# Squares of the last stage on ScalarE, an input mixed in place four quads earlier, and VectorE's sums ahead of its preparation steps

## The chip, the cores and the metric

One core of a Trainium2 chip. The metric is the device time of one execution in microseconds, median of several runs; lower is better. The engines are TensorE (PE in the profile), VectorE (DVE), ScalarE (ACT), GpSimd (POOL) and SyncE (SP), which here only issues DMAs. Each works through its own instructions in order and waits on semaphores.

## The reference

Three layers over a batch of 2, a sequence of 768 and a width of 512, in fp32. The first is a windowed attention with block summaries. The other two are these:

```python
# second layer
xt = x.transpose(0, 2, 1)
h = np.maximum(xt @ w_tok1, 0.0) @ w_tok2
u = x + h.transpose(0, 2, 1)
x = u + np.maximum(u @ w_ch1, 0.0) @ w_ch2      # w_ch1: 512 x 1536
# third layer (the last stage of the kernel)
x_prev = x shifted by one row of the sequence, zeros first
xk = mu_k * x + (1.0 - mu_k) * x_prev
xr = mu_r * x + (1.0 - mu_r) * x_prev
k = np.maximum(xk @ w_k, 0.0)                    # w_k: 512 x 1024
v = k * k @ w_v
r = 1.0 / (1.0 + np.exp(-(xr @ w_r)))
out = r * v
```

## The kernel before, in words

Each fp32 factor is split into a high part (fp32r) and a low part, the rest; three matmuls (high x high, high x low, low x high) make one product (`three`, L1311 to L1313). The high part is a copy by ScalarE or GpSimd, the low part a subtraction by VectorE or GpSimd. Activations lie transposed in `u`: four tiles of 128 channels, and per batch one zero column and 768 columns, so that `x_prev` is the same tile read one column earlier (`u_tile(kk, g, 1)`).

**Quads.** The channel products are cut into quads of 256 x 256 blocks of the weight and two halves (384 columns) of the sequence, done with seven products in place of eight (`PRODUCTS`, in the order P1, P6, P2, P7, P5, P4, P3) on sums and differences of the blocks of the weight (`w1S`, by GpSimd) and of the activation (`ucF`). There are 20 quads: 0 to 5 and 6 to 11 for the two batches of the second layer (`quad`), 12 to 15 and 16 to 19 for the two batches of the last stage (`quad_k`). A set is the activation of one batch and layer; set 3 feeds quads 16 to 19.

**PE** runs for quad q: P1, two value tiles of quad q-1, P6, one tile, P2, two, P7, one, P5, two, P4, two, P3, two (`TILE_GAPS`; a value tile is k*k @ w_v for 128 rows). The first value tile needs the low part of R21 of quad q-1, the seventh that of R12. P1 waits until all five sums of the quad before are done and its weights are split; P7 waits for the sum of P6, P4 for that of P7, P3 for that of P5.

**VectorE** makes five sums per quad (`plus`, L1177: P6 into u2, P7 into u3, P5 into c22, P4 into c21, P3 into c12), the squares (L1194 for `kr`, L1181 for the other three: max with 0, times itself), the low parts of the results (`low_k`, L1187) and of the next quad's weights (`low_w1`, L997, L1000 and L1003), and what `ahead(q, place)` lists for one of three places in the quad. **ScalarE** turns out P1 (`p1`, L812), relu of P2 (`kr`, L818), the high parts of the weights (`high_w1`), of the results (`high_k`, L809), and its share of `ahead`. **GpSimd** makes the sums of weights (L568 to L573, waiting for the last product of the quad before), splits w_v (L578, L582) and the low part of w_r (L587).

**What `ahead` does** is written out by hand in tables, keyed by quad and place: `T_AT` and `U_AT` make the sums and the high (L716) and low parts of the next set, `MIX_AT` mixes xk, `XR_AT` mixes xr (ScalarE (1 - mu) * x_prev, L751, then VectorE adds mu * x, L1075), `XR_HIGH_AT` and `XR_LOW_AT` split it (L757, L1082). A mix or split works on 128 x 384.

**The gates.** After the products of quad 16, PE computes xr @ w_r for batch 0 in six tiles (`gate(0)`), after quad 19 that of batch 1; ScalarE applies the sigmoid (L838), VectorE multiplies by v (L1234). The gate's first three tiles need the low parts of xr tiles 0 to 3, the others those of 4 to 7, and `wait_piece` both halves of w_r.

## Time and profile before

| | |
|---|---|
| median of 3 runs | 509.79 us (508.15 to 510.85) |
| profiled execution | 510.17 us, its span 508.4 us |
| mean granted clock of TensorE | 0.977 of full speed |
| busy: PE, PEld, DVE, ACT, POOL | 92%, 82%, 70%, 45%, 43% of the span |
| chain that ended last | PE 69%, DVE 15%, ACT 7%, idle issue 5% |

The span runs from the first to the last instruction; the time of a run holds 1.77 us more. Times in rows are microseconds from the span's start. A row of a timeline is one instruction (or a few alike, with their count), in brackets how long its engine stood idle before it and what released it. A row of windows gives the busy time in one stretch and TensorE's mean granted clock there, 1.00 for 2.4 GHz and 0.50 for 1.2 GHz.

### The profile page before, as it was taken

To read this page: it belongs to the slowest core of one execution; us is meant where nothing else is said; L and a number is where in the kernel's file an instruction comes from. 1 tells how busy PE (TensorE), PEld (TensorE's weight loads), DVE (VectorE), ACT (ScalarE), POOL (GpSimd) and SP (SyncE) were. 2 spreads that over 40 slices of the span, in tenths; PEclk is the share of its full clock that TensorE was granted. 3 is DMA by queue.
4 is the path that set the end of the run, shared out by engine and by line. 5 is a ranking of instruction groups with operands and counts; after the bars stand their busy time and mean duration, and the time that the engine had idled before them with its cause. 6 is when DMAs were issued, how large, how long until landed. Compare 5 with 4: busy or idle time off the path is not lost.

```text
span 508.4 us, 7788 instructions
## 1 busy us (share of the span) xinstructions
PE 466.3 (92%) x2848; PEld 415.3 (82%) x2848; DVE 354.1 (70%) x732; ACT 228.9 (45%) x473; POOL 220.9 (43%) x213
## 2 busy tenths in 40 slices
PE   5789889999999999999999999697898759989997
PEld 4677778889999999999998998586787648878885
DVE  6589996496766565567676863876987993699503
ACT  6699996464333333334433343161264542552120
POOL 6647765422534566433564346516245290063000
PEclk9899999999999999999999999998989959999999
DMA  6999944311121121221212212112020312210003
GB/s 183 244 227 224 197 94 81 111 41 43 42 85 58 67 84 41 84 79 46 85 44 81 63 62 83 43 43 77 8 82 1 124 41 104 104 43 0 2 0 124
DMA packets 45441, 41.20 MB, mean 81 GB/s; under 512 B 20832, under 2 KB 36704, under 8 KB 45408
## 3 DMA queue, kind: packets, MB, share of 16 engines
q1 hardware_dynamic: 45408, 40.78, 29.5%
q8 instruction: 19, 0.31, 0.3%
q14 instruction: 14, 0.11, 0.1%
HBM read 37.62 MB, written 3.15 MB: 80 GB/s over the span
## 4 chain that ended last, share of the span: by engine, by line
PE 69%; DVE 15%; ACT 7%; issue 5%; DMA 2%; POOL 2%; SPq 0%; ACTq 0%; DVEq 0%; POOLq 0%
PE bank L1311 16%; PE bank L1312 15%; PE bank L1313 15%; PE bank L1448 12%; PE bank L1449 6%; ACT e_sb L638 3%; DVE rL L1187 2%; DMA v<-in_v_dram 2%; DVE xrL L1082 2%; DVE c L1181 2%; DVE w1L L1003 2%; ACT qbd L618 1%; PE bank L1291 1%; DVE c L1177 1%; PE bank L1363 1%
## 5 line engine op out<-in xcount | busy, mean ns | idle before, releaser
L1311 PE MATMUL bank<-ucH,w1H 128*128 128x384 f32 x280 | 96.1, 343 | 13.7 <-DVE c L1177 8.5
L1313 PE MATMUL bank<-ucH,w1L 128*128 128x384 f32 x280 | 95.0, 339 | 0.0
L1312 PE MATMUL bank<-ucL,w1H 128*128 128x384 f32 x280 | 94.9, 339 | 0.0
L568 POOL TENSOR_TENSOR w1S<-stg 128x256 f32<-128x256 f32 x20 | 19.8, 991 | 168.9 <-PE bank L1313 168.9
L1311 PEld LDWEIGHTS bank<-ucH,w1H 128*128 128x128 f32 x280 | 53.2, 190 | 22.6 <-issue 15.6
L582 POOL TENSOR_TENSOR w2L<-stg,w2H 128x512 fp32r<-128x512 f32 x40 | 60.2, 1526 | 1.6
L1312 PEld LDWEIGHTS bank<-ucL,w1H 128*128 128x128 f32 x280 | 53.6, 191 | 2.0
L1313 PEld LDWEIGHTS bank<-ucH,w1L 128*128 128x128 f32 x280 | 53.3, 190 | 0.0
L774 ACT ACTIVATE rH<-c 128x384 fp32r<-128x384 f32 x36 | 18.9, 526 | 68.4 <-DVE c L1115 68.4
L809 ACT ACTIVATE rH<-c 128x384 fp32r<-128x384 f32 x24 | 12.6, 525 | 61.2 <-DVE c L1181 61.2
L1312 PE MATMUL bank<-w2L,rH 128*128 128x512 f32 x96 | 38.8, 404 | 0.0
L1311 PE MATMUL bank<-w2H,rH 128*128 128x512 f32 x96 | 38.7, 404 | 0.0
L1313 PE MATMUL bank<-w2H,rL 128*128 128x512 f32 x96 | 38.6, 402 | 0.0
L1448 PE MATMUL bank<-rL,w2H 128*128 128x512 f32 x96 | 37.6, 392 | 0.0
L1448 PE MATMUL bank<-rH,w2L 128*128 128x512 f32 x96 | 37.6, 392 | 0.0
L1448 PE MATMUL bank<-rH,w2H 128*128 128x512 f32 x96 | 37.6, 392 | 0.0
L1115 DVE TENSOR_TENSOR u<-bank,p 128x384 f32<-128x384 f32 x24 | 13.4, 557 | 33.1 <-PE bank L1313 33.0
L578 POOL CAST w2H<-stg 128x1024 fp32r<-128x1024 f32 x20 | 21.9, 1096 | 28.9 <-PE bank L1313 25.3
L1120 DVE SCALAR_TENSOR_TENSOR rL<-c,rH 128x384 fp32r<-128x384 f32 x36 | 23.7, 659 | 13.6 <-ACT rH L774 13.6
L638 ACT ACTIVATE e_sb<-s_sb,nmx 128x120 f32<-128x120 f32 x96 | 29.8, 384 | 0.8 <-DVE nmx L902 0.8
L1311 PE MATMUL bank<-WrH,xrH 128*128 128x512 f32 x48 | 19.8, 411 | 9.3 <-DVE xrL L1082 9.3
L1449 PE MATMUL bank<-rH,w2L 128*128 128x256 f32 x96 | 27.0, 281 | 0.0
(142 smaller groups left out, 1187.5 us busy)
## 6 DMA issues: line engine op xcount, KB each, us to landing
stg<-in_moe_w_ch_dram SPq DMA_DIRECT2D x24, 512.0 KB, 3.5
stg<-in_moe_w_k_dram SPq DMA_DIRECT2D x8, 512.0 KB, 3.5
stg<-in_moe_w_v_dram SPq DMA_DIRECT2D x8, 512.0 KB, 3.4
vw<-in_v_dram SPq DMA_DIRECT2D x16, 240.0 KB, 5.6
kn<-in_k_dram SPq DMA_DIRECT2D x8, 384.0 KB, 5.6
qn<-in_q_dram SPq DMA_DIRECT2D x8, 384.0 KB, 6.7
v<-in_v_dram SPq DMA_DIRECT2D x8, 384.0 KB, 5.6
stg<-in_moe_w_tok_dram SPq DMA_DIRECT2D x6, 256.0 KB, 3.9
```

Source lines behind the costliest of these rows:

```text
L568: pool.tensor_tensor(s1, a21, a22, ALU.add).then_inc(w1s_done, 1)
L578: pool.tensor_copy(hi, stg[2][:, :]).then_inc(wb_high, 1)
L582: pool.tensor_tensor(lo[:, part], stg[2][:, part], hi[:, part].bitcast(F32), ALU.subtract).then_inc(wb_split, 1)
L638: act.activation(e_sb[par][:, n, :], s_sb[r][:, n, :], ACT.Exp, bias=nmx[:, r, n:n + 1], scale=-1.0).then_inc(exp_done, 1)
L774: act.activation(rH[slot][:, f, half * GR:half * GR + GR], src, func).then_inc(rh_done, 1)
L1115: dve.tensor_tensor(dst[:, :], acc, other[:, :], ALU.add).then_inc(sum_done, 1)
L1120: dve.scalar_tensor_tensor(out=rL[slot][:, f, half * GR:half * GR + GR], in0=src, scalar=0.0, in1=hi.bitcast(F32), op0=ALU.max, op1=ALU.su ...
L1311: pe.matmul(dst, wH, mH, start=start, stop=False, **more)
L1312: pe.matmul(dst, wH, mL, start=False, stop=False, **more)
L1313: return pe.matmul(dst, wL, mH, start=False, stop=stop, **more)
L1448: pe.matmul(wide, w, r[slot][:, f, 0:512], start=begin, stop=end, skip_group_check=True)
L1449: ins = pe.matmul(side, w, r[slot][:, f, 512:S], start=begin and d % 2 == 0, stop=end, skip_group_check=True)
```

## The change

In the last stage the squares go from VectorE to ScalarE. `kr` is squared by an ACTIVATE in place right after its relu, and its high part is made next, ahead of `high_w1`. For R22, R21 and R12 a new `power` waits for VectorE's sum, then does Relu in place, waits for that, and does Square in place; `high_k` follows. VectorE's `square` and its product for `kr` are gone.

xr of batch 0 is mixed in quads 8 to 11, one of its eight tiles at each of places 1 and 2, half 1 of the sequence first. It overwrites `u`, which nothing else needs by then; ScalarE's part goes through the two buffers `sg`. Its splits follow in quad 16, one or two tiles per place, the last four after it. For batch 1 mixes and splits go one per place in quads 17 to 19. `MIX_AT` of quad 13 and `U_AT` of quads 14 and 15 are spread over more places.

In VectorE's `quad_k` the order changes: `low_w1` part 0 ahead of `low_k(R11)`, P4's sum ahead of `low_k(R22)`, P3's sum ahead of `low_k(R21)`, place 3 ahead of `low_k(R12)`.

```diff
--- before.py
+++ after.py
@@ -220,7 +220,7 @@
         tk_mixed, xk_mixed = sem("tk_mixed"), sem("xk_mixed")
         tr_mixed, xr_mixed = sem("tr_mixed"), sem("xr_mixed")
         xrh_done, xrl_done = sem("xrh_done"), sem("xrl_done")
-        kr_done, sq_done, v_done, tile_done = sem("kr_done"), sem("sq_done"), sem("v_done"), sem("tile_done")
+        kr_done, relu_done, sq_done, v_done, tile_done = sem("kr_done"), sem("relu_done"), sem("sq_done"), sem("v_done"), sem("tile_done")
         wr_done, sg_done, o_done = sem("wr_done"), sem("sg_done"), sem("o_done")
         ld_out = [sem("ld_out0"), sem("ld_out1"), sem("ld_out2")]
 
@@ -312,13 +312,17 @@
                 (9, 1): (3, 4), (9, 2): (5, 6), (14, 1): (3, 4), (14, 2): (5, 6)}
         U_AT = {(1, 1): (0,), (2, 1): (1,), (3, 1): (3,), (4, 1): (4,), (4, 2): (5,), (5, 1): (6,), (5, 2): (2,),
                 (10, 1): (0, 1), (10, 2): (3,), (11, 1): (4, 5), (11, 2): (6, 2),
-                (14, 3): (0, 1), (15, 1): (3, 4), (15, 2): (5, 6), (15, 3): (2,)}
+                (14, 3): (0,), (15, 1): (1, 3), (15, 2): (4, 5), (15, 3): (6, 2)}
 
         MIX_AT = {(7, 1): ((0, 0), (1, 0)), (7, 2): ((2, 0), (3, 0)), (8, 1): ((0, 1), (1, 1)), (8, 2): ((2, 1), (3, 1)),
-                  (13, 1): ((0, 0), (1, 0), (2, 0), (3, 0)), (13, 2): ((0, 1), (1, 1), (2, 1), (3, 1))}
-        XR_AT = {(16, 1): (0, 1), (16, 2): (2, 3), (17, 1): (0, 1), (17, 2): (2, 3), (18, 1): (4, 5), (18, 2): (6, 7)}
-        XR_HIGH_AT = {(16, 2): (0, 1), (16, 3): (2, 3), (17, 2): (0, 1), (17, 3): (2, 3), (18, 2): (4, 5), (18, 3): (6, 7)}
-        XR_LOW_AT = {(16, 3): (0, 1, 2, 3), (17, 3): (0, 1, 2, 3), (18, 3): (4, 5, 6, 7)}
+                  (13, 1): ((0, 0), (1, 0), (2, 0)), (13, 2): ((3, 0), (0, 1), (1, 1)), (13, 3): ((2, 1), (3, 1))}
+
+        XR_ORDER = (4, 5, 6, 7, 0, 1, 2, 3)
+        XR_AT = {(8, 1): (4,), (8, 2): (5,), (9, 1): (6,), (9, 2): (7,), (10, 1): (0,), (10, 2): (1,), (11, 1): (2,),
+                 (11, 2): (3,), (17, 1): (0,), (17, 2): (1,), (17, 3): (2,), (18, 1): (3,), (18, 2): (4,), (18, 3): (5,),
+                 (19, 1): (6,), (19, 2): (7,)}
+        XR_SPLIT_AT = {(16, 1): (0,), (16, 2): (1, 2), (16, 3): (3,), (17, 2): (0,), (17, 3): (1,), (18, 1): (2,),
+                       (18, 2): (3,), (18, 3): (4,), (19, 1): (5,), (19, 2): (6,), (19, 3): (7,)}
 
         def set_ahead(q):
             return 1 if q < NFP else 2 if q < NQ else 3
@@ -748,13 +752,21 @@
 
             def mix_r(b, n):
                 kk, half = n % KT, n // KT
-                act.activation(xrF[:, kk, half * GR:half * GR + GR], u_tile(kk, 2 * b + half, 1), ACT.Copy,
+                if b == 0:
+                    i = XR_ORDER.index(n)
+                    if i >= 2:
+                        act.wait_ge(xr_mixed, i - 1)
+                    dst = sg[i % 2][:, 0:GR]
+                else:
+                    dst = xrF[:, kk, half * GR:half * GR + GR]
+                act.activation(dst, u_tile(kk, 2 * b + half, 1), ACT.Copy,
                                scale=omu[:, 1, kk:kk + 1]).then_inc(tr_mixed, 1)
 
             def high_xr(b, n):
                 kk, half = n % KT, n // KT
-                act.wait_ge(xr_mixed, 8 * b + n + 1)
-                act.activation(xrH[:, kk, half * GR:half * GR + GR], xrF[:, kk, half * GR:half * GR + GR],
+                part = slice(half * GR, half * GR + GR)
+                act.wait_ge(xr_mixed, 8 if b == 0 else 8 + n + 1)
+                act.activation(xrH[:, kk, part], u_tile(kk, half) if b == 0 else xrF[:, kk, part],
                                ACT.Copy).then_inc(xrh_done, 1)
 
             def ahead(q, place):
@@ -764,7 +776,7 @@
                     high_u(set_ahead(q), i)
                 for n in XR_AT.get((q, place), ()):
                     mix_r(q // 17, n)
-                for n in XR_HIGH_AT.get((q, place), ()):
+                for n in XR_SPLIT_AT.get((q, place), ()):
                     high_xr(q // 17, n)
 
             def quad(q):
@@ -804,9 +816,16 @@
 
                 slot, done, k = q % 2, NPROD * q, q - NQ
 
-                def high_k(n, f, half, src):
+                def high_k(n, f, half, c):
                     act.wait_ge(sq_done, 4 * k + n)
-                    act.activation(rH[slot][:, f, half * GR:half * GR + GR], src[:, :], ACT.Copy).then_inc(rh_done, 1)
+                    act.activation(rH[slot][:, f, half * GR:half * GR + GR], c[:, :], ACT.Copy).then_inc(rh_done, 1)
+
+                def power(n, c):
+
+                    act.wait_ge(sum_done, 5 * q + n + 1)
+                    act.activation(c[:, :], c[:, :], ACT.Relu).then_inc(relu_done, 1)
+                    act.wait_ge(relu_done, 3 * k + n - 1)
+                    act.activation(c[:, :], c[:, :], ACT.Square).then_inc(sq_done, 1)
 
                 act.wait_ge(prod_done, done + P1)
                 act.activation(p1[:, :], bank[0][:, 0:GR], ACT.Copy).then_inc(p1_done, 1)
@@ -816,15 +835,20 @@
                 act.wait_ge(prod_done, done + P2)
                 act.wait_ge(rl_done, 4 * (q - 1) + R11)
                 act.activation(kr[:, :], bank[0][:, 0:GR], ACT.Relu).then_inc(kr_done, 1)
+                wait_second(act, q - 2)
+                act.wait_ge(kr_done, k + 1)
+                act.activation(kr[:, :], kr[:, :], ACT.Square).then_inc(sq_done, 1)
+                high_k(R11, 0, 0, kr)
                 if q < NA - 1:
                     high_w1(q + 1)
-                wait_second(act, q - 2)
-                high_k(R11, 0, 0, kr)
                 ahead(q, 2)
+                power(R22, c22)
                 high_k(R22, 1, 1, c22)
                 if q == 16:
                     high_wr(1)
+                power(R21, c21)
                 high_k(R21, 1, 0, c21)
+                power(R12, c12)
                 high_k(R12, 0, 1, c12)
                 ahead(q, 3)
 
@@ -849,8 +873,6 @@
                     act.wait_ge(x2_done, 6 * B)
                 quad_k(q)
                 if q == NQ + NKP:
-                    for n in range(KT, 2 * KT):
-                        mix_r(0, n)
                     for n in range(KT, 2 * KT):
                         high_xr(0, n)
                     gates(0)
@@ -1070,17 +1092,23 @@
 
             def mix_r(b, n):
                 kk, half = n % KT, n // KT
-                dst = xrF[:, kk, half * GR:half * GR + GR]
-                dve.wait_ge(tr_mixed, 8 * b + n + 1)
-                dve.scalar_tensor_tensor(out=dst, in0=u_tile(kk, 2 * b + half), scalar=mu[:, 1, kk:kk + 1], in1=dst,
+                x = u_tile(kk, 2 * b + half)
+                if b == 0:
+                    i = XR_ORDER.index(n)
+                    dst, part = x, sg[i % 2][:, 0:GR]
+                else:
+                    i, dst = n, xrF[:, kk, half * GR:half * GR + GR]
+                    part = dst
+                dve.wait_ge(tr_mixed, 8 * b + i + 1)
+                dve.scalar_tensor_tensor(out=dst, in0=x, scalar=mu[:, 1, kk:kk + 1], in1=part,
                                          op0=ALU.mult, op1=ALU.add).then_inc(xr_mixed, 1)
 
             def low_xr(b, n):
                 kk, half = n % KT, n // KT
                 part = slice(half * GR, half * GR + GR)
                 dve.wait_ge(xrh_done, 8 * b + n + 1)
-                dve.tensor_tensor(xrL[:, kk, part], xrF[:, kk, part], xrH[:, kk, part].bitcast(F32),
-                                  ALU.subtract).then_inc(xrl_done, 1)
+                dve.tensor_tensor(xrL[:, kk, part], u_tile(kk, half) if b == 0 else xrF[:, kk, part],
+                                  xrH[:, kk, part].bitcast(F32), ALU.subtract).then_inc(xrl_done, 1)
 
             def ahead(q, place):
                 for kk, half in MIX_AT.get((q, place), ()):
@@ -1091,7 +1119,7 @@
                     low_u(set_ahead(q), i)
                 for n in XR_AT.get((q, place), ()):
                     mix_r(q // 17, n)
-                for n in XR_LOW_AT.get((q, place), ()):
+                for n in XR_SPLIT_AT.get((q, place), ()):
                     low_xr(q // 17, n)
 
             def wide(b, d):
@@ -1176,11 +1204,6 @@
                     dve.wait_ge(prod_done, done + n)
                     dve.tensor_tensor(dst[:, :], acc, other[:, :], ALU.add).then_inc(sum_done, 1)
 
-                def square(n, c):
-                    dve.wait_ge(sum_done, 5 * q + n + 1)
-                    dve.scalar_tensor_tensor(out=c[:, :], in0=c[:, :], scalar=0.0, in1=c[:, :], op0=ALU.max,
-                                             op1=ALU.mult).then_inc(sq_done, 1)
-
                 def low_k(n, f, half, src):
                     hi = rH[slot][:, f, half * GR:half * GR + GR]
                     dve.wait_ge(rh_done, 4 * q + n)
@@ -1190,38 +1213,33 @@
                 dve.wait_ge(p1_done, q + 1)
                 dve.wait_ge(sum_done, 5 * q)
                 plus(P6, u2, Bk, p1)
-                dve.wait_ge(kr_done, k + 1)
-                dve.tensor_tensor(kr[:, :], kr[:, :], kr[:, :], ALU.mult).then_inc(sq_done, 1)
                 ahead(q, 1)
                 if q == NQ:
                     wide(1, 0)
                 plus(P7, u3, Bk, p1)
-                low_k(R11, 0, 0, kr)
                 if q < NA - 1:
                     low_w1(q + 1, 0)
+                low_k(R11, 0, 0, kr)
                 dve.wait_ge(sum_done, 5 * q + 2)
                 dve.wait_ge(rl_done, 4 * q)
                 plus(P5, c22, A, u3)
-                square(R22, c22)
                 ahead(q, 2)
                 if q == NQ:
                     wide(1, 1)
+                plus(P4, c21, Bk, p1)
                 low_k(R22, 1, 1, c22)
-                plus(P4, c21, Bk, p1)
-                square(R21, c21)
                 if q < NA - 1:
                     low_w1(q + 1, 1)
-                low_k(R21, 1, 0, c21)
                 if q == NQ:
                     side(1, 1)
                 plus(P3, c12, A, u2)
-                square(R12, c12)
-                low_k(R12, 0, 1, c12)
+                low_k(R21, 1, 0, c21)
                 if q == NQ:
                     wide(1, 2)
                     wide(1, 3)
                     side(1, 3)
                 ahead(q, 3)
+                low_k(R12, 0, 1, c12)
 
             def outputs(b):
                 for st in range(NT):
@@ -1242,8 +1260,6 @@
                     dve.wait_ge(x2_done, 6 * B)
                 quad_k(q)
                 if q == NQ + NKP:
-                    for n in range(KT, 2 * KT):
-                        mix_r(0, n)
                     for n in range(KT, 2 * KT):
                         low_xr(0, n)
                     outputs(0)
```

## Rows read from the trace of the kernel before

**Rows 1.** Windows: length, busy PE PEld DVE ACT POOL, clock, DMA

```profile
308.20:328.70 20.50, 16.14 (x90) 14.60 (x91) 11.37 (x19) 4.65 (x9) 10.09 (x10) 1.00 0.18 58
328.70:349.30 20.60, 17.45 (x79) 15.39 (x79) 17.05 (x28) 8.79 (x17) 7.80 (x8) 0.91 0.13 45
349.30:369.00 19.70, 17.41 (x79) 15.35 (x79) 13.59 (x21) 4.74 (x9) 7.59 (x6) 0.92 0.17 53
369.00:387.70 18.70, 17.43 (x78) 15.17 (x78) 17.27 (x23) 9.03 (x15) 8.00 (x6) 0.91 0.16 53
387.70:413.00 25.30, 15.96 (x79) 14.06 (x79) 21.12 (x28) 13.48 (x25) 13.63 (x11) 0.88 0.25 83
413.00:431.50 18.50, 18.50 (x73) 15.10 (x74) 11.03 (x13) 6.37 (x10) 5.68 (x5) 0.88 0.17 65
431.50:447.20 15.70, 15.70 (x80) 13.91 (x78) 10.63 (x20) 7.67 (x15) 1.20 (x2) 1.00 0.26 93
447.20:464.50 17.30, 16.02 (x79) 13.86 (x79) 16.61 (x25) 8.43 (x17) 7.00 (x6) 1.00 0.09 31
```

**Rows 2.** Timeline of PE (start, us; idle before, releaser), quads 12, 13

```profile
320.22 0.41 PE L1311 MATMUL bank<-ucH,w1H 128*128 128x384 f32 x1 [1.34 <-DVE u L1177]
...
328.73 0.66 PE L1311 MATMUL bank<-ucH,w1H 128*128 128x384 f32 x1 [3.05 <-DVE c L1177]
```

**Rows 3.** Timeline of DVE, end of quad 13

```profile
344.37 0.55 DVE L1177 TENSOR_TENSOR c<-bank,p 128x384 f32<-128x384 f32 x1
344.95 1.04 DVE L1181 SCALAR_TENSOR_TENSOR c<-c 128x384 f32<-128x384 f32 x1
345.92 1.75 DVE L1003 TENSOR_TENSOR w1L<-w1S,w1H 128x1024 fp32r<-128x1024 f32 x1
347.59 1.07 DVE L1187 TENSOR_TENSOR rL<-c,rH 128x384 fp32r<-128x384 f32 x1
348.58 0.54 DVE L1177 TENSOR_TENSOR c<-bank,u 128x384 f32<-128x384 f32 x1
```

**Rows 4.** Timeline of POOL, same stretch

```profile
346.54 1.71 POOL L571 TENSOR_TENSOR w1S<-w1S,stg 128x256 f32<-128x256 f32 x1
```

**Rows 5.** Timelines of DVE, ACT, DVE, POOL in quad 17

```profile
435.25 0.56 DVE L1177 TENSOR_TENSOR u<-bank,p 128x384 f32<-128x384 f32 x1 [2.21 <-PE bank L1313]
...
436.89 0.49 ACT L818 ACTIVATE kr<-bank 128x384 f32<-128x384 f32 x1 [2.68 <-PE bank L1313]
...
444.38 0.56 DVE L1181 SCALAR_TENSOR_TENSOR c<-c 128x384 f32<-128x384 f32 x1
...
446.00 1.15 POOL L568 TENSOR_TENSOR w1S<-stg 128x256 f32<-128x256 f32 x1 [27.16 <-PE bank L1313]
```

**Rows 6.** Groups by line on ACT (busy, mean ns | idle before)

```profile
L716 ACT ACTIVATE ucH<-ucF 128x768 fp32r<-128x768 f32 x22 | 17.7, 836 | 3.3 <-DVE u L1040 3.1
...
L809 ACT ACTIVATE rH<-c 128x384 fp32r<-128x384 f32 x24 | 12.6, 525 | 61.2 <-DVE c L1181 61.2
...
L751 ACT ACTIVATE xrF<-u,omu 128x384 f32<-128x384 f32 x16 | 8.8, 602 | 0.0
...
L838 ACT ACT_TABLE_LOAD x1 | 1.3, 1283 | 0.0
```

**Rows 7.** Timelines of POOL and DVE, quad 16 and behind it

```profile
400.30 2.40 POOL L587 TENSOR_TENSOR WrL<-stg,WrH 128x1024 fp32r<-128x1024 f32 x1 [6.97 <-ACT WrH L724]
...
400.75 2.37 DVE L1181 SCALAR_TENSOR_TENSOR c<-c 128x384 f32<-128x384 f32 x1
...
407.67 5.14 DVE L1082 TENSOR_TENSOR xrL<-xrF,xrH 128x384 fp32r<-128x384 f32 x4
```

**Rows 8.** Timelines of DVE and PE, end of quad 9

```profile
273.28 1.22 DVE L1003 TENSOR_TENSOR w1L<-w1S,w1H 128x1024 fp32r<-128x1024 f32 x1
274.41 1.11 DVE L1120 SCALAR_TENSOR_TENSOR rL<-c,rH 128x384 fp32r<-128x384 f32 x1
...
276.13 0.41 PE L1311 MATMUL bank<-ucH,w1H 128*128 128x384 f32 x1 [0.76 <-DVE c L1115]
```

## Prediction

> **What bounds the kernel now.** I read the windows of the last stage first, one window from the start of one quad's products to the next [rows 1]: in this program TensorE is the bound, and the question is where it isn't fed. Quad 17 is the clean one: 15.70 us, PE busy in all of it, clock 1.00. Every other quad of the stage should take the same, and takes more: 20.50 (12), 20.60 (13), 19.70 (14), 18.70 (15), 25.30 (16, to the gate), 17.30 (18). The gate of batch 0 takes 18.50 at a mean clock of 0.88.
>
> The timeline of PE shows the holes [rows 2]: PE stands still 1.34 us inside quad 12 and 3.05 us before the first product of quad 13. The others come from [rows 1], length less PE's busy time: 3.15 before quad 14, 2.29 before 15, 1.27 before 16, 9.3 before the gate (25.30 - 15.96) and 1.3 in quad 18 (17.30 - 16.02). There is a second loss: in quads 13 to 15 PE is busy 17.4 us for 15.7 us of work, at a mean clock of 0.91 to 0.92. After the holes of 3.05, 3.15, 2.29 and 9.3 us the clock drops to its half level (1.2 GHz) for a while; after those of 1.34, 1.27 and 1.3 it doesn't. So a long hole costs its length and some 1.6 us more.
>
> What PE waits for is named in [rows 2]: `c` of L1177, VectorE's sum `plus(P3, c12)`. The timeline of DVE at the end of quad 13 [rows 3] shows why it is late: between the sum of P4 (344.37) and that of P3 (348.58) stand a square of 1.04, `low_w1` part 1 of 1.75 and `low_k(R21)` of 1.07. In this stretch GpSimd works [rows 4], and the two inputs from SBUF make DVE's operations wait for it: without GpSimd `low_w1` part 1 takes 1.22 [rows 8] and the square 0.56 [rows 5].
>
> For the clocking of a quad I use quad 17 [rows 5]: its first product starts at 431.45 (431.5 in [rows 1]); P6's sum starts at +3.80, P2's relu at +5.44, and GpSimd, which waits for P3, at +14.55. Between P6 and P2 stands one value tile: 5.44 - 3.80 = 1.64 for a product and a tile. From P2 to P3 come three products with two tiles and one with one, so two tiles and a product take (14.55 - 5.44 - 1.64) / 3 = 2.49. P7, P5, P4, P3 end at +7.9, 9.6, 12.1, 14.5, and the next quad wants c12 at about +15.6.
>
> **Part 1: squares to ScalarE.** DVE loses four operations per quad, 0.56 each [rows 5], more where one waits for GpSimd (1.04 in [rows 3]): 2.2 us or more. ACT gains seven: four squares and three relus (the relu of `kr` exists). No Square runs before; the nearest row is ACT's copy of the same tile, 525 ns [rows 6]; bounds are 0.49 (the relu from PSUM [rows 5]) and 0.60 (L751, with a pointer operand). No row has an ACT operation that waits for the one before it on ACT; DVE's `plus` to square is 0.58 from start to start in [rows 3] for a sum of 0.55, so I take 0.03 for the wait: 0.56 each, 3.9 per quad. ACT's queue per quad becomes: p 0.4, kr with square and copy 1.6, `high_w1` 1.8, three times relu, square, copy 1.65 = 5.0, in sum 8.8; with 8 mixes of 0.55 (8.8 over 16) in quad 13 13.2; with 6 high parts of u (17.7 over 22, 0.8 each) in quad 15 13.6, of 15.7 [rows 6]. It holds.
>
> The new queue, quad 13, offsets from its first product. ACT: p, three mixes to 3.2; kr 5.44 to 7.0; `high_w1` to 8.75; mixes to 10.3; R22 (c22 is there at 10.4) to 12.1; R21 (c21 at 12.7) to 14.4; R12 (c12 at 15.15) to 16.8; two mixes to 17.8. DVE: P6 4.3, mixes 5.9, P7 8.4, w1 part 0 9.4, R11 9.85, P5 10.35, mixes 11.95, P4 12.6, R22 13.1, w1 part 1 14.25 (GpSimd starts at 14.55, so the price is the clean 1.22), P3 14.55 to 15.1. That is before 15.6: no hole. Late instead are R12 and the mixes behind it, done at about +18.9; its reader, the seventh value tile of the next quad, comes at +25. R21's reader, the first value tile, comes at +16.8, and R21 is low at 15.6 to 16.2: half a microsecond of cover; that is what is late next.
>
> **Part 2: order of sums and preparation.** The high and low parts of set 3 are spread (14.3 to 15.3), so quad 15 has six. There GpSimd stands against DVE until +7 and I get P4's sum at 14.1 instead of 12.6, P3's at 16.2 to 16.8: a hole of 0.9, quad 15 16.6 us (bounds 15.7 and 17.7). Quad 12 keeps its 1.34, since `wide(1, 0)` still stands ahead of P7's sum. After it, counted from P4's start at 320.22 [rows 2]: `wide(1, 1)` waits for the chunk behind P4 (+2.4, at 322.6, 0.6 us), P4's sum ends at 323.7, R22 at 324.2, w1 part 1 at 325.4 to 325.9, `side(1, 1)` at 326.5, P3's sum at about 327; the square of 0.5 to 1 us and `low_k(R21)` of 1.07 that stood there are gone. Quad 13 starts at 326.9 instead of 328.7. The hole is 1.2, of the size after which the clock stayed. Quad 12: 18.7.
>
> **Part 3: xr of batch 0 in quads 8 to 11.** This takes eight mixes out of quad 16 and the stretch after it. Before, the gate's first tile waited for four `low_xr` of 5.14 us together, behind `low_k(R12)` and behind squares of which one took 2.37 while GpSimd's `WrL` (2.40) ran [rows 7]. After, three of four are done inside the quad. The last waits: c12 at 15.15 to 17.1 (as GpSimd's second `WrL` goes after or before w1 part 1), R12 on ACT 1.7, `high_xr(3)` 0.4, `low_xr(3)` 0.55: the gate starts at 17.9 to 19.8; I take 19.0 for 25.3. A hole of 3 us remains, hence the half clock for one stretch: the gate's work is 18.5 x 0.88 = 16.3 at full clock, I take 17.9 (bounds 16.3 and 18.5). Batch 1: mixes and splits go one per place; the four `low_xr` that stood ahead of P6's sum in quad 18 are gone: 15.7 for 17.3.
>
> The price is in quads 8 to 11: one mix (some 0.55 on ACT and on DVE, like their other operations on 384 columns) at two places each. Behind place 1 DVE waits for P7 anyway. Place 2 stands ahead of the sums of P4 and P3, and DVE is at the edge there: before quad 10 PE already stands 0.76, behind a `low_r(R21)` of 1.11 for 0.55 [rows 8]. Pushed by half a microsecond, w1 part 1 also slides under GpSimd. I count 0.55, 0.8, 0.4 and 0.75: 2.5 us lost (bounds 0.5, if a wait for GpSimd absorbs the mix, and 4.2, if each adds one more GpSimd operation of about 1 us at two of them). No DMA moves: SP waits for the same splits, at nearly the same offsets.
>
> **Sum**, quads 12, 13, 14, 15, 16, gate, 17, 18: before 20.5 + 20.6 + 19.7 + 18.7 + 25.3 + 18.5 + 15.7 + 17.3 = 156.3; after 18.7 + 15.7 + 15.7 + 16.6 + 19.0 + 17.9 + 15.7 + 15.7 = 135.0. That is 21.3 less, 2.5 back: 18.8. The profiled execution took 510.17 for a span of 508.4, so 491.4; that execution lies 0.4 above the median of the runs, 509.79: 491.0. Own range by the bounds: 2.0 + 0.9 + 1.1 + 1.6 down gives 485.4; 1.7 + 1.1 + 0.8 + 0.6, and 1.6 for a clock that falls before quad 13, gives 496.8 up.
>
> **A rule against it.** The rows say: relu and multiply cost VectorE one operation of 0.56 [rows 5], ScalarE two of about 0.53 [rows 6]. The Trainium skill (ScalarE: Activation LUTs, Rules for kernel authors) puts relu and mul on VectorE, not ScalarE. By that rule the move loses; the trace agrees with it on engine time, but ACT is busy 4.7 to 9.0 us of quads 13 to 15 and DVE 13.6 to 17.3 [rows 1].
>
> **Rivals.**
> 1. The longer chain takes the sum's place. DVE is in order, and `low_k(R22)`, which now waits for three ACT steps, stands ahead of w1 part 1 and of P3's sum. There is 0.5 us between ACT's 12.1 and DVE's 12.6, and 0.3 more before P3. For it: ACT comes out of its mixes only at 10.3, when c22 is there. If a square with its wait costs 1 us more than I take, quads 13 to 16 lose some 1 to 1.5 us each with half clock after one or two: 8 us of the gain gone, 499 (497 to 503). Chance 0.15.
> 2. On the other side: Square and Relu (or Copy) are in different tables. A load takes 1.28 us [rows 6]. With two loads per square, 8 x 1.28 = 10.3 per quad on ACT, 13.6 + 10.3 = 23.9 for a quad of 15.7: 8.2 x 8 = 66 us on top of 491, some 555. It decides once ACT's queue is 18.8 / 8 = 2.4 longer than 15.7, 4.5 us above 13.6: four loads per quad. Against it: Exp, Sigmoid, Relu and Copy run with two loads in all, one of them before the first Exp. Chance 0.03.
> 3. The engine-time rule above as a mechanism: ACT gains 3.9 where DVE loses 2.2; if that chain set the quad's length, 1.7 x 8 = 14 us slower than 510, 524. It needs the first value tile to wait for R21 in all quads. Against it: R21 has 0.5 us of cover. Chance 0.02.
> 4. The change doesn't reach the holes, because the quads 8 to 11 and contention with GpSimd give the gain back: DVE is busy 13.6 to 17.3 us of quads 13 to 15 now and keeps 11 of them. Two waits for GpSimd per quad at 1 us each, 500 to 508 with the clock. Chance 0.05.
>
> **Chances.** Forecast 0.75, the others as given. The range takes in the forecast's own 485.4 to 496.8 and reaches to rival 1's 499 and a little: 484.5 to 500.5. A run here can tell 0.5% (2.5 us) from no change. Faster: 0.75 + 0.15 + 0.04 = 0.94; within 0.5% 0.01; slower 0.05.
>
> **What would show it.** Right: first products of quads 14 to 16 with no hole of over 1 us; clock 1.00 from quad 13 to 16; the gate's hole about 3 us, released by `xrL`; DVE's sum of P3 directly behind `w1L`; ACT in rows relu, square, copy of about 0.53 without idle between them; one table load besides the first. New holes of 0.5 to 1.5 us before quads 9 to 12. Wrong: the value line waiting for rL, a Square of another duration than a copy, table loads in the stage, or the clock at half where PE was fed.

## The result and the profile after

The changed kernel takes 488.48 us (median of 4 runs, 486.57 to 489.74), the kernel before 509.49 in the same comparison: a ratio of 0.9584, 95% interval 0.9543 to 0.9625. Forecast were 491.0 in a range of 484.5 to 500.5. The profiled execution of the changed kernel is its fastest run, 486.57, with a span of 484.8 us. One of the ten runs of a1 below took 758.54 us at a mean clock of 0.562 and is left out of its ratio.

Windows of the changed kernel from one quad's first product to the next one's, for quads 12 to 16, the gate of batch 0, and quads 17 and 18. The columns are those of [rows 1]: start and end, length, busy time of PE, PEld, DVE, ACT, POOL (instructions), granted clock, DMA.

```profile
309.20:328.10 18.90, 16.12 (x90) 14.62 (x90) 8.84 (x15) 7.54 (x15) 8.06 (x8) 1.00 0.17 55
328.10:343.90 15.80, 15.76 (x78) 14.17 (x79) 13.86 (x22) 12.01 (x24) 6.03 (x7) 1.00 0.22 72
343.90:359.60 15.70, 15.70 (x80) 14.05 (x79) 13.92 (x19) 9.29 (x18) 7.58 (x8) 1.00 0.18 62
359.60:375.30 15.70, 15.70 (x80) 14.07 (x79) 13.74 (x18) 12.30 (x23) 8.50 (x8) 1.00 0.22 67
375.30:393.10 17.80, 15.80 (x79) 13.84 (x78) 13.74 (x19) 15.01 (x28) 8.11 (x5) 1.00 0.19 62
393.10:409.60 16.50, 16.47 (x72) 13.55 (x73) 5.68 (x10) 5.22 (x9) 10.00 (x10) 1.00 0.40 133
409.60:425.30 15.70, 15.70 (x79) 14.07 (x78) 8.52 (x15) 9.54 (x19) 1.12 (x2) 1.00 0.27 94
425.30:441.00 15.70, 15.70 (x79) 14.05 (x78) 12.51 (x19) 11.22 (x23) 6.44 (x6) 1.00 0.09 34
```

Against [rows 1]: quads 13, 14, 15 and 18 are at the clean length with PE busy throughout; the clock is 1.00 in every window. ACT's busy time in quad 13 has risen from 8.79 to 12.01 of 15.8, DVE's fell from 17.05 of 20.6 to 13.86. What is left of the holes, in PE's timeline:

```profile
275.85 0.41 PE L1327 MATMUL bank<-ucH,w1H 128*128 128x384 f32 x1 [1.44 <-DVE c L1143]
...
309.24 0.41 PE L1327 MATMUL bank<-ucH,w1H 128*128 128x384 f32 x1 [1.39 <-issue]
...
321.25 0.41 PE L1327 MATMUL bank<-ucH,w1H 128*128 128x384 f32 x1 [1.34 <-DVE u L1205]
...
328.14 0.41 PE L1327 MATMUL bank<-ucH,w1H 128*128 128x384 f32 x1 [1.44 <-DVE c L1205]
...
393.13 0.47 PE L1327 MATMUL bank<-WrH,xrH 128*128 128x512 f32 x1 [2.02 <-DVE xrL L1110]
```

The first two (before quads 10 and 12) were 0.76 [rows 8] and 0.52 and have grown by 0.68 and 0.87 us: the price of the mixes in quads 8 to 11. The gate's hole is 2.02 us in place of 9.3. DVE at the end of quad 13, where [rows 3] had 4.2 us from the sum of P4 to that of P3:

```profile
340.27 0.56 DVE L1205 TENSOR_TENSOR c<-bank,p 128x384 f32<-128x384 f32 x1 [0.17 <-PE bank L1329]
340.75 0.55 DVE L1210 TENSOR_TENSOR rL<-c,rH 128x384 fp32r<-128x384 f32 x1
341.21 1.22 DVE L1025 TENSOR_TENSOR w1L<-w1S,w1H 128x1024 fp32r<-128x1024 f32 x1
342.71 0.56 DVE L1205 TENSOR_TENSOR c<-bank,u 128x384 f32<-128x384 f32 x1 [0.28 <-PE bank L1329]
```

Both sums now wait for PE, and `w1L` takes its clean 1.22: it is done at 342.43, and GpSimd starts at 342.76. And the chain on ACT for R21, three steps that follow one another:

```profile
340.87 0.53 ACT L826 ACTIVATE c<-c 128x384 f32<-128x384 f32 x1 [0.67 <-DVE c L1205]
341.42 0.53 ACT L828 ACTIVATE c<-c 128x384 f32<-128x384 f32 x1
341.98 0.53 ACT L821 ACTIVATE rH<-c 128x384 fp32r<-128x384 f32 x1
```

A Square lasts as long as a copy, and from start to start 0.55 to 0.56 us.

### The profile page after: what moved, and what is told of

The parts are those of the page before. It is cut to its first block, busy times and chain, and to the rows that moved or that the text cites. A ratio compares the mean times of both kernels' runs of the same rounds, so it can differ in the third digit from the quotient of the medians.

```text
span 484.8 us, 7812 instructions
## 1 busy us (share of the span) xinstructions
PE 459.0 (95%) x2848; PEld 410.3 (85%) x2848; DVE 331.2 (68%) x700; ACT 258.2 (53%) x529; POOL 217.3 (45%) x213
## 4 chain that ended last, share of the span: by engine, by line
PE 74%; ACT 9%; DVE 6%; issue 5%; DMA 2%; POOL 2%; SPq 0%; ACTq 0%; DVEq 0%; POOLq 0%
PE bank L1327 18%; PE bank L1329 18%; PE bank L1328 18%; PE bank L1464 12%; PE bank L1465 6%; ACT e_sb L642 4%; DMA v<-in_v_dram 2%; ACT qbd L622 2%; DVE ucF L1056 1%; ACT kt L630 1%; DVE w1L L1025 1%; POOL xL L546 1%; DVE rL L1148 1%; DVE c L1143 1%; PE bank L1397 1%
## 5 line engine op out<-in xcount | busy, mean ns | idle before, releaser
L1327 PE MATMUL bank<-ucH,w1H 128*128 128x384 f32 x280 | 94.7, 338 | 6.0 <-DVE c L1143 1.7
L1329 PE MATMUL bank<-ucH,w1L 128*128 128x384 f32 x280 | 94.0, 336 | 0.0
L572 POOL TENSOR_TENSOR w1S<-stg 128x256 f32<-128x256 f32 x20 | 17.9, 894 | 148.7 <-PE bank L1329 148.7
L586 POOL TENSOR_TENSOR w2L<-stg,w2H 128x512 fp32r<-128x512 f32 x40 | 58.9, 1494 | 1.6
L786 ACT ACTIVATE rH<-c 128x384 fp32r<-128x384 f32 x36 | 18.9, 526 | 69.4 <-DVE c L1143 69.4
L582 POOL CAST w2H<-stg 128x1024 fp32r<-128x1024 f32 x20 | 22.8, 1142 | 30.2 <-PE bank L1329 24.3
L1035 DVE TENSOR_TENSOR ucL<-ucF,ucH 128x768 fp32r<-128x768 f32 x22 | 24.9, 1157 | 3.7 <-ACT ucH L720 3.7
L1465 PE MATMUL bank<-rL,w2H 128*128 128x256 f32 x96 | 26.9, 280 | 0.0
```

The costliest lines, as they stand in the source:

```text
L582: pool.tensor_copy(hi, stg[2][:, :]).then_inc(wb_high, 1)
L586: pool.tensor_tensor(lo[:, part], stg[2][:, part], hi[:, part].bitcast(F32), ALU.subtract).then_inc(wb_split, 1)
L786: act.activation(rH[slot][:, f, half * GR:half * GR + GR], src, func).then_inc(rh_done, 1)
L1035: dve.tensor_tensor(ucL[b % 2][:, i, :, :], src, ucH[b % 2][:, i, :, :].bitcast(F32), ALU.subtract).then_inc(ul_done, 1)
L1327: pe.matmul(dst, wH, mH, start=start, stop=False, **more)
L1329: return pe.matmul(dst, wL, mH, start=False, stop=stop, **more)
```

## The experiments

Each was compared with the kernel before on the same chip. The groups a, b and c ran on three chips, on which the kernel before took 509.49, 510.49 and 510.41, so a difference between medians of two groups is uncertain by about 1 us. Firmer are the distances between first products in the profiles: quads 8 to 11 take 64.3 to 64.5 us in every kernel that leaves them as they were or mixes behind P3's sum. The time to the first product of quad 8, ahead of which nothing was changed, is 242.3 to 244.2. The table of distances stands behind the first four.

**a1, VectorE's order alone.** The squares stay where they were, each right behind its sum.

```diff
                 plus(P7, u3, Bk, p1)
-                low_k(R11, 0, 0, kr)
                 if q < NA - 1:
                     low_w1(q + 1, 0)
+                low_k(R11, 0, 0, kr)
...
-                low_k(R22, 1, 1, c22)
                 plus(P4, c21, Bk, p1)
                 square(R21, c21)
+                low_k(R22, 1, 1, c22)
...
-                low_k(R21, 1, 0, c21)
...
                 plus(P3, c12, A, u2)
                 square(R12, c12)
-                low_k(R12, 0, 1, c12)
+                low_k(R21, 1, 0, c21)
...
                 ahead(q, 3)
+                low_k(R12, 0, 1, c12)
```

> The kernel before with VectorE's new order alone; the squares stay on VectorE, each right behind its sum, and the xr tables stay. Theory: the holes before quads 13 to 16 come from what stands between P4's and P3's sum, and taking low_k(R22) and low_k(R21) out of the way is enough for most of them: about 498 us (500 at worst), the 9.3 us hole before the gate stays. Rival (only the four squares taken off VectorE count): 506 or more.

Measured: 507.47 us, ratio 0.9952 (0.9926 to 0.9978). The theory failed: the order alone is worth 2 us (3.0 in the table below), not 11.

**a2, squares alone.** ScalarE's `quad_k` of the changed kernel, VectorE's of before without its squares.

```diff
                 plus(P6, u2, Bk, p1)
-                dve.wait_ge(kr_done, k + 1)
-                dve.tensor_tensor(kr[:, :], kr[:, :], kr[:, :], ALU.mult).then_inc(sq_done, 1)
...
-                square(R22, c22)
...
-                square(R21, c21)
...
-                square(R12, c12)
```

> The kernel before with the squares on ScalarE alone; VectorE's order and the xr tables stay. Theory: VectorE has 0.56 to 1 us less ahead of P3's sum, but low_k(R21) still stands before it and waits for the three steps on ScalarE; holes of under 0.7 us stay, no half clock: about 495 us. Rival 1 of the prediction (the longer chain takes the sum's place): the holes stay at 2 to 3 us, 503 or more.

Measured: 502.01 us, ratio 0.9848 (0.9808 to 0.9887). Between the theory (495) and rival 1 (503), and nearer to the rival.

**a3, xr and the tables.** The changed kernel with the `quad_k` of before on both engines. With xr come the spread `MIX_AT` and `U_AT` of quads 13 to 15; no run parts them from xr.

> The kernel before with xr of batch 0 in place in quads 8 to 11 and the new tables alone; squares and VectorE's order stay. Theory: the gate's hole falls from 9.3 to about 3 us and quad 18 loses its 1.3, quads 8 to 11 cost 2.5, holes before quads 13 to 16 stay: about 504 us. Rival (the price in quads 8 to 11 eats it): 507 or more.

Measured: 503.1 us, ratio 0.9876 (0.9838 to 0.9914). Near the 504 expected, but not by the way expected: the holes before quads 13 to 16 were to stay, and the one before quad 14 fell from 3.13 to 1.07 us. No operation of xr stands in quads 13 to 15 in either kernel, so these quads' 4.9 us come from the spread tables, in part through a half clock that stayed away. The gate's hole is 4.71 us, not 3. PE's timeline before quad 14:

```profile
349.26 0.41 PE L1325 MATMUL bank<-ucH,w1H 128*128 128x384 f32 x1 [1.07 <-DVE c L1193]
```

**a4, squares and order, without xr.** The kernel before with both engines' `quad_k` of the changed one; all tables are those of before.

> The changed kernel without the xr part: squares on ScalarE and VectorE's new order, with the old xr tables. Theory: quads 13 to 16 at 15.7 to 16.6, gate's hole still 5 us or more: about 494 us, that is 5 to 6 above the changed kernel and no more than 2 below squares alone. Rival (the xr part gives nothing): 489.

Measured: 488.04 us, ratio 0.9572 (0.9531 to 0.9613). The rival was right: beside the other two parts, xr and the tables give nothing (the changed kernel 488.48).

Microseconds between first products, worked out from PE's timelines; "gate" is the length of batch 0's gate, "sum" goes from quad 12 to the end of quad 18:

| | 8 to 11 | 12 | 13 | 14 | 15 | 16 | gate | 17 | 18 | sum |
|---|---|---|---|---|---|---|---|---|---|---|
| before | 64.5 | 20.5 | 20.5 | 19.7 | 18.8 | 25.2 | 18.5 | 15.7 | 17.3 | 156.3 |
| a1, order | 64.5 | 20.5 | 20.1 | 18.9 | 17.9 | 24.1 | 18.7 | 15.7 | 17.4 | 153.3 |
| a2, squares | 64.3 | 20.0 | 18.7 | 16.4 | 17.1 | 23.8 | 19.2 | 16.3 | 16.9 | 148.3 |
| a3, xr and tables | 66.8 | 20.5 | 18.5 | 18.4 | 17.2 | 20.6 | 18.7 | 15.7 | 15.9 | 145.6 |
| a4, squares and order | 64.5 | 18.9 | 15.8 | 15.7 | 15.9 | 18.9 | 18.0 | 15.7 | 15.7 | 134.5 |
| changed, all three | 66.9 | 18.9 | 15.8 | 15.7 | 15.7 | 17.9 | 16.5 | 15.7 | 15.7 | 131.8 |

Why the order alone does so little is seen in DVE's timeline of a1 at the end of quad 13 (first product at 328.83):

```profile
344.44 0.55 DVE L1177 TENSOR_TENSOR c<-bank,p 128x384 f32<-128x384 f32 x1
345.02 0.56 DVE L1181 SCALAR_TENSOR_TENSOR c<-c 128x384 f32<-128x384 f32 x1
345.50 1.10 DVE L1187 TENSOR_TENSOR rL<-c,rH 128x384 fp32r<-128x384 f32 x1
346.52 1.74 DVE L1003 TENSOR_TENSOR w1L<-w1S,w1H 128x1024 fp32r<-128x1024 f32 x1
348.19 0.54 DVE L1177 TENSOR_TENSOR c<-bank,u 128x384 f32<-128x384 f32 x1
```

P4's sum itself is late, at +15.6 and without waiting for PE (PE itself is some 1.7 us late here by a stretch at half clock, as in the kernel before: busy 17.45 for 15.70 [rows 1]); in the changed kernel it waits for PE and starts at +12.1. So `w1L` falls into GpSimd's time and takes 1.74 for 1.22. Where the queue falls behind is seen earlier in the same timeline:

```profile
336.80 0.56 DVE L1194 TENSOR_TENSOR kr<-kr 128x384 f32<-128x384 f32 x1 [1.61 <-ACT kr L818]
337.28 2.20 DVE L1068 SCALAR_TENSOR_TENSOR ucF<-u,mu,ucF 128x384 f32<-128x384 f32 x4
339.40 0.55 DVE L1177 TENSOR_TENSOR u<-bank,p 128x384 f32<-128x384 f32 x1
```

VectorE stands idle 1.61 us at the product for `kr`, which needs P2's relu, and the four mixes of place 1 and P7's sum stand behind it. From here on no sum of the quad waits for PE. With the squares on ScalarE the mixes come first and fill that idle time (in the changed kernel P7's sum waits 1.47 us for PE). Whether `ahead(q, 1)` put ahead of the product for `kr`, with all squares left on VectorE, would give part of this was not run. An order can't mend a queue that is behind before the place of the edit, and a1's edit begins behind P7's sum. With the squares alone P7's sum waits for PE (1.41 us) and `w1L` is clean again, and another wait takes over:

```profile
343.21 0.55 DVE L1189 TENSOR_TENSOR c<-bank,p 128x384 f32<-128x384 f32 x1
343.68 1.22 DVE L1015 TENSOR_TENSOR w1L<-w1S,w1H 128x1024 fp32r<-128x1024 f32 x1
345.47 1.12 DVE L1199 TENSOR_TENSOR rL<-c,rH 128x384 fp32r<-128x384 f32 x1 [0.58 <-ACT rH L809]
346.52 0.54 DVE L1189 TENSOR_TENSOR c<-bank,u 128x384 f32<-128x384 f32 x1
```

`low_k(R21)` waits 0.58 us for ACT's third step and then takes 1.12 us for 0.55, with GpSimd at work from 344.66, and P3's sum stands behind it. That is rival 1 of the prediction, in the kernel without the new order. Two more runs split the order.

**c2 and c3, squares and one move of the order.** Cut, against a2:

```diff
c2:
-                low_k(R21, 1, 0, c21)
                 if q == NQ:
                     side(1, 1)
                 plus(P3, c12, A, u2)
+                low_k(R21, 1, 0, c21)
c3:
-                low_k(R22, 1, 1, c22)
                 plus(P4, c21, Bk, p1)
+                low_k(R22, 1, 1, c22)
```

> Squares on ScalarE alone, and of the new order only P3's sum ahead of low_k(R21). Theory: what kept the holes with the squares alone was low_k(R21) waiting in VectorE's queue for ScalarE's three steps, in front of P3's sum; moving that one operation gives nearly all of what the whole order gives: about 489 (487 to 491), against 502 for the squares alone and 488 for the whole order. Rival (P4's sum behind low_k(R22) counts as much): 495.

> Squares on ScalarE alone, and of the new order only P4's sum ahead of low_k(R22). Theory: P4's sum comes half a microsecond earlier and so does R21's chain, but low_k(R21) still waits ahead of P3's sum; most holes stay: 498 to 502. Rival (P4's sum counts as much): 495.

Measured: c2 490.78 us, ratio 0.9600 (0.9560 to 0.9641); c3 498.7, ratio 0.9766 (0.9725 to 0.9808). Of the 14 us between the squares alone (502.0) and the whole order (488.0), moving P3's sum ahead of `low_k(R21)` gives 11.2. Moving P4's alone gives 3.3. These are medians of two chips; from quad 12 to the end of quad 18 the profiles give 10.0 (138.3) and 3.7 (144.6) of 13.8.

**b1, the mixes at place 3.**

```diff
-        XR_AT = {(8, 1): (4,), (8, 2): (5,), (9, 1): (6,), (9, 2): (7,), (10, 1): (0,), (10, 2): (1,), (11, 1): (2,),
-                 (11, 2): (3,),
+        XR_AT = {(8, 3): (4, 5), (9, 3): (6, 7), (10, 3): (0, 1), (11, 3): (2, 3),
```

> The changed kernel with the eight mixes of xr of batch 0 at place 3 of quads 8 to 11, behind P3's sum, two per quad, in place of one at each of places 1 and 2. Theory: the 2.4 us that quads 8 to 11 lost are the mixes' place ahead of P4's and P3's sums, where VectorE has no slack; behind P3's sum it idles 2.4 us. The holes of 1.44 before quad 10 and 1.39 before quad 12 fall to those of the kernel before (0.76, 0.52): 2.4 less than the changed kernel, about 486. Rival (the mixes cost wherever they stand, by contention with GpSimd, which is at work there): no difference, or slower.

Measured: 486.20 us, ratio 0.9521 (0.9491 to 0.9551), 2.3 less than the changed kernel. Quads 8 to 11 take 64.5 again, and the hole before quad 10 is 0.76 as in [rows 8]. The price was the place, not the mixes: the pair there takes long beside GpSimd too (2.40 for two), but no sum stands behind it.

```profile
259.82 2.40 DVE L1103 SCALAR_TENSOR_TENSOR u<-u,mu,sg 128x384 f32<-128x384 f32 x2
```

**b2, the second layer's last additions one sum later.**

```diff
-                if q == NQ:
-                    wide(1, 0)
                 plus(P7, u3, Bk, p1)
...
                 if q == NQ:
-                    wide(1, 1)
+                    wide(1, 0)
                 plus(P4, c21, Bk, p1)
+                if q == NQ:
+                    wide(1, 1)
...
+                plus(P3, c12, A, u2)
                 if q == NQ:
                     side(1, 1)
-                plus(P3, c12, A, u2)
```

> The changed kernel with the additions wide(1,0), wide(1,1) and side(1,1) of quad 12 one sum later each, so that no sum waits behind a second-layer chunk. Theory: the hole of 1.34 before P4 of quad 12 goes, and that of 1.44 before quad 13 falls below 0.5: 2 to 2.5 less than the changed kernel, about 486. Rival (PE waits for something else there, such as the sum of P6 or the splits): under 1 us.

Measured: 485.81 us, ratio 0.9516 (0.9484 to 0.9547), 2.7 less than the changed kernel. Both holes of quad 12 are gone: 15.7 for 18.9. The three moves were made together; of them only `wide(1, 0)` stood ahead of P7's sum, for which P4 waited, while the share of each in the hole before quad 13 is not parted.

**b3, xr tile 3 split at place 2 of quad 16.**

```diff
-        XR_SPLIT_AT = {(16, 1): (0,), (16, 2): (1, 2), (16, 3): (3,),
+        XR_SPLIT_AT = {(16, 1): (0,), (16, 2): (1, 2, 3),
```

> The changed kernel with the split of xr tile 3 at place 2 of quad 16 in place of place 3, so that the gate waits for no step behind R12. Theory: the gate's hole of 2.02 (released by xrL) falls to about 0.7, then set by GpSimd's second WrL; in runs where that hole brings a stretch at half clock, 1.5 more: about 486. Rival (WrL or P3's sum was nearly as late): under 0.5 us.

Measured: 485.81 us, ratio 0.9522 (0.9494 to 0.9550), 2.7 less. The first matmul of the gate:

```profile
391.86 0.50 PE L1327 MATMUL bank<-WrH,xrH 128*128 128x512 f32 x1 [0.68 <-POOL WrL L591]
```

The hole is 0.68, and its releaser is now GpSimd's second `WrL`, as expected: 1.34 us of the 2.7. The rest stays open. Three of the changed kernel's four runs have a mean clock of 0.996, as b1's profiled execution has with one stretch at half clock in the gate (last section). But c1's profiled execution has 0.996 too, and its half clock (0.53 in the window 19.2 to 22.8 us) lies far ahead of the gate.

**b4, each relu of `power` done twice.**

```diff
                     act.activation(c[:, :], c[:, :], ACT.Relu).then_inc(relu_done, 1)
-                    act.wait_ge(relu_done, 3 * k + n - 1)
+                    act.wait_ge(relu_done, 2 * (3 * k + n - 1) - 1)
+                    act.activation(c[:, :], c[:, :], ACT.Relu).then_inc(relu_done, 1)
+                    act.wait_ge(relu_done, 2 * (3 * k + n - 1))
```

> The changed kernel with the relu of R22, R21 and R12 done twice, 0.56 us more on each chain and 1.7 per quad on ScalarE's queue (13.3 us more in the stage); the result is the same. Theory: the chain has about 0.5 us of cover before VectorE reads R22 and R21, so it costs at most 1.5 us in sum: 489 to 490. Rival 1 of the prediction (the chain is what sets the sums): 0.5 to 0.6 per quad and the clock, 493 or more.

Measured: 491.89 us, ratio 0.9629 (0.9593 to 0.9666): 3.4 more than the changed kernel, more than twice the 1.5 I allowed, and less than the rival's 4.5. In the profile quads 12, 14, 16 and 18 are 0.6 to 0.9 longer, 2.8 together, quads 13, 15 and 17 are unchanged, and the gate is 1.5 longer at half clock behind a hole of 2.95. In quad 14 PE waits in the middle of the quad, for the sum of P6, and DVE's timeline shows why:

```profile
347.67 2.94 DVE L1092 SCALAR_TENSOR_TENSOR ucF<-u,mu,ucF 128x384 f32<-128x384 f32 x2 [2.12 <-ACT ucF L750]
350.54 1.65 DVE L1212 TENSOR_TENSOR rL<-c,rH 128x384 fp32r<-128x384 f32 x1
352.10 0.55 DVE L1207 TENSOR_TENSOR u<-bank,p 128x384 f32<-128x384 f32 x1
```

The two mixes of quad 13's place 3 stand on ACT behind the chain for R12; VectorE waits 2.12 us for them, then takes 2.94 us for two mixes and 1.65 for a low part, and the next quad's first sum stands behind them. The cover that ends first is there, not at R21.

**c1, b1 to b3 together.**

> The changed kernel with all three edits that each gained: xr mixes at place 3 of quads 8 to 11, the wide and side additions of quad 12 one sum later, the split of xr tile 3 at place 2 of quad 16. Theory: they touch different holes, so they add: 2.4 + 3.2 + 1.4 by their pitches, and no hole of 2 us is left that could bring the half clock (about 1 us on the median of the changed kernel's runs): about 480.5 (479 to 482). Rival (the holes hide one another, as the parts of the change did): 483 or more.

Measured: 480.65 us (479.75 to 480.98), ratio 0.9402 (0.9372 to 0.9432): 7.8 us less than the changed kernel. The three edits add, since each closes holes that no other touches: in the profiles, from quad 8 to the end of quad 18, 2.4, 3.0 and 1.4 alone (b1's longer gate at half clock left out) and 6.8 together. Its windows for quad 12, quad 16 and the gate:

```profile
308.10:323.80 15.70, 15.70 (x91) 14.63 (x91) 10.22 (x16) 8.43 (x17) 7.51 (x7) 1.00 0.18 61
...
371.10:387.60 16.50, 15.82 (x80) 13.86 (x78) 13.21 (x18) 14.13 (x26) 8.09 (x5) 1.00 0.19 65
387.60:404.10 16.50, 16.50 (x73) 13.62 (x74) 6.13 (x11) 6.10 (x11) 9.99 (x10) 1.00 0.38 135
```

## Why the prediction was right, and where it wasn't

The sum was near and somewhat low: 18.8 us forecast, 21.0 measured between medians, 23.6 between the profiled spans. Of the 23.6, 1.4 lie before quad 8 (its first product at 242.3 for 243.7), where nothing was changed. From quad 8 to the end of quad 18 it is 22.1: quad 15 gave 0.9 more than forecast, quad 16 1.1 and the gate 1.4. The queues of parts 1 and 2 came out as worked out; what part 3 put down to xr in quads 16 and 18 came from the other two parts (6), so the near sum doesn't bear out how it was split.

1. **Part 1, the costs on ScalarE**: right. The new operations last 0.526 us on average (taken 0.53) and 0.56 with their wait. The 0.03 for the wait was too small, though: copies of the same tile that don't wait for one another start 0.41 to 0.42 apart (`xrH` in the kernel before), so the wait takes 0.14 to 0.15 of the queue. No table is loaded for Square: two loads in all, so rival 2 is out. Rival 3, the engine-time rule, needed value tiles that wait for R21; none does in the changed kernel, and it takes 488, not 524. The squares alone (a2) already gain 7.5 us.
2. **Part 1, quads 13 to 15**: 20.6 + 19.7 + 18.7 were to become 15.7 + 15.7 + 16.6 and became 15.8 + 15.7 + 15.7. The step that was too dear is quad 15: I had DVE's P4 sum done at +14.1, since GpSimd would hold up every low part of u. It starts at +12.3 (371.88 - 359.59) and is done at +12.8: the two low parts at place 1 took 3.54 us together and P7's sum stood at +8.2.
3. **Why the holes close**: half right. I worked out the new queue as a whole and it holds to 0.1 us (P4's sum starts at +12.1, P3's at +14.6). But the prediction told squares and order as two savings on one line, and didn't see the 1.61 us that VectorE idles at the product for `kr`. The runs show that neither alone does it (2 and 7.5 us), and both together 21.5: the squares bring the queue back to PE's pace, the order takes the wait for the longer chain out of it.
4. **Rival 1**: it is real without the new order (a2: 502). With it, its price is 3.4 us for 0.56 us more per chain (b4), where it had 8 for 1. I named R21's reader as what is late next; it is the sum of P6, behind the mixes of place 3. Rival 4 had VectorE keep 11 us of its work in quads 13 to 15; it keeps 13.7 to 13.9, and they still take 15.7 to 15.8.
5. **Part 2, quad 12**: 18.7 forecast, 18.9 measured, its 1.34 kept, the hole before quad 13 at 1.44 (forecast 1.2) and no half clock behind it. The cause named for the 1.34, `wide(1, 0)` ahead of P7's sum, agrees with b2.
6. **Part 3, the gate**: the number was near (17.9 for 19.0, the low bound), by luck, since the attribution was wrong. I put the 6.3 us of quad 16 and the 1.6 of quad 18 down to xr. Squares and order alone bring quad 16 from 25.2 to 18.9, the gate's hole from 9.3 to 3.06, and quad 18 to 15.7 (a4). The four `low_xr` of 5.14 us [rows 7] were not too much work but late work, in GpSimd's time. GpSimd in the kernel before, and VectorE in a4 with the same four operations, still at place 3 (which now stands ahead of `low_k(R12)`), where GpSimd has nothing to do between 390.45 and 394.03:

```profile
407.42 3.00 POOL L582 TENSOR_TENSOR w2L<-stg,w2H 128x512 fp32r<-128x512 f32 x2
```

```profile
390.79 1.95 DVE L1094 TENSOR_TENSOR xrL<-xrF,xrH 128x384 fp32r<-128x384 f32 x4
```

Beside the other parts, xr and the tables give 1.0 in quad 16, 0.2 in quad 15 and, in the profiled runs, 1.5 on the gate's clock, and take 2.4 in quads 8 to 11: nothing in sum. On the kernel before they give 6.4 (a3), and only in part by xr: of the 10.7 us between first products of quads 12 and 19, 4.9 lie in quads 13 to 15, where the tables were spread.
7. **Part 3, quads 8 to 11**: 2.5 forecast, 66.9 - 64.5 = 2.4 measured, and by its cause (b1). By quad it was 0, 1.1, 0.4 and 1.0 for 0.55, 0.8, 0.4 and 0.75.
8. **The clock**: I counted 1.6 us for a stretch at half clock in the gate. The profiled execution has none (16.5), but it is the fastest of four; the others show a mean clock of 0.996 for 0.999 and take 488.3 to 489.7, and where their clock fell is not known. The median lies 2.5 us below the forecast, the profiled execution 4.8 below the 491.4 forecast for it.

## What to carry to other kernels

When several edits aim at one in-order queue, work out where the queue is late before each: an edit behind that point gives little until the lateness is gone (2 us here), and then the parts give more together than the sum of each alone, or a part gives nothing more. Look for it at an operation that idles for another engine with ready work behind it, as the product for `kr` did. Lateness also has a price of its own here, since VectorE's work that slips into GpSimd's time took 2.6 and 4.2 times as long (5.14 us for 1.95, 2.37 for 0.56). Moved work should go behind the last result that the bounding engine waits for (place 3), not just to a quad with spare time; and after each gain, the next hole is named by the same view: here three small moves were worth another 7.8 us.

## What the runs showed of the hardware

The length of a hole does not alone decide whether TensorE's clock falls. The changed kernel and b1 have the same hole before the gate; b1's timeline:

```profile
391.41 0.47 PE L1327 MATMUL bank<-WrH,xrH 128*128 128x512 f32 x1 [2.03 <-DVE xrL L1110]
```

With 2.02 us the gate ran at 1.00 and took 16.5; with 2.03 us this is its window (length, busy PE to POOL, clock):

```profile
391.40:409.50 18.10, 18.09 (x73) 14.77 (x74) 5.67 (x10) 5.21 (x9) 9.98 (x10) 0.91 0.34 120
```

The same work takes 18.1 us. And in a3 a longer hole before quad 15 left the clock at 1.00, while the 2.29 us of the kernel before at this place [rows 1] brought it down; PE's timeline and the window of a3:

```profile
367.61 0.41 PE L1325 MATMUL bank<-ucH,w1H 128*128 128x384 f32 x1 [2.44 <-DVE c L1193]
```

```profile
367.60:384.80 17.20, 15.93 (x78) 13.97 (x78) 15.35 (x22) 8.30 (x14) 8.01 (x6) 1.00 0.17 57
```

In the profiles of all kernels here, of the holes in the last stage those of 1.44 us or less never brought the half clock, those of 2.95 or more always did, and those from 2.0 to 2.5 four times and five times not. What decides among these no run here shows. For a single run it makes some 1.5 us. The prediction's rule "a long hole costs its length and some 1.6 us more" fits holes of about 3 us: the gate, 16.5 us at full clock, took 18.0 behind 2.95 and 3.06. Behind holes of 3.75 to 9.29 us it took 18.3 to 19.2, so 1.8 to 2.7 more. And one run of a4 that wasn't profiled has a mean clock of 1.000, though a4's profile shows 3.06 us before the gate; so "always" holds for the profiled executions alone.

VectorE's operations with two inputs from SBUF took longer while GpSimd was at work, as foreseen (a low part 1.12 us for 0.55 in a2); the reverse I had not priced. GpSimd's second `WrL` took 3.47 us where it started together with VectorE's `w1L` of 1.22. It took 2.40 in the kernel before [rows 7], and 3.19 in a4, where the last 0.94 us of `w1L` ran beside it: that is 1.07 and 0.79 more, a little less than `w1L` still had to run (1.21 and 0.94). DVE and POOL of the changed kernel:

```profile
388.25 1.22 DVE L1025 TENSOR_TENSOR w1L<-w1S,w1H 128x1024 fp32r<-128x1024 f32 x1
```

```profile
388.26 3.47 POOL L591 TENSOR_TENSOR WrL<-stg,WrH 128x1024 fp32r<-128x1024 f32 x1 [6.46 <-ACT WrH L728]
```
